# A maximum over partitions taken on another engine, the sums of a weight moved ahead of one tile, and four loads moved behind a loop

## What is computed

```python
# 1: 4 sequences, 8 heads, 768 steps, head size 64: a decaying state
state = gamma * state + outer(k[t], v[t]);  y[t] = scale * q[t] @ state
# 2: x is y as (3072, 512); phi has 32 columns (slots), 4 of them for each of 8 experts
logits = x @ phi
d = softmax(logits, axis=0)              # over the 3072 rows: a maximum and a sum by column
slot_in = (d.T @ x).reshape(8, 4, 512)
slot_out[e] = relu(slot_in[e] @ w1[e]) @ w2[e]
x2 = softmax(logits, axis=1) @ slot_out
# 3: x2 (3072, 512): each row goes to its two best of 8 experts
out[rows] += weight * (relu(x2[rows] @ w1b[e]) @ w2b[e])
```

## Time and profile before

| | |
|---|---|
| median of 3 runs | 539.45 us (538.11 to 540.13) |
| the profiled execution | 539.68 us, its span 537.8 us |
| busy in the span | PE 492.4 us, PEld 291.5, DVE 276.2, ACT 185.8, POOL 254.2 |
| DMA | 107.93 MB, mean 201 GB/s |
| chain that ended last | PE 76%, DMA 13%, DVE 3%, issue 3% |

### The profile page before, as it was taken

The page is one execution under the profiler, slowest core; times in us unless marked ns, Lnnn a source line. Parts: engine busy times, 40 slices in busy tenths (PEclk is TensorE's granted clock), DMA queues, the critical chain, the costliest instruction groups (busy, mean ns, idle before and its releaser), DMA issues.

```text
span 537.8 us, 13565 instructions
## 1 busy us (share of the span) xinstructions
PE 492.4 (92%) x4844; PEld 291.5 (54%) x4845; DVE 276.2 (51%) x443; ACT 185.8 (35%) x346; POOL 254.2 (47%) x217
## 2 busy tenths in 40 slices
PE   3999999987978667989999999999999999999995
PEld 3877787863567243444544544545545445445452
DVE  2676766666221897463646455464545332433422
ACT  0222222221003537665455363554442222223210
POOL 2222222202000024525777868786878766666553
PEclk9999999998997889999999999999999999999999
DMA  7999999989999999342466342132232332433410
GB/s 276 400 359 398 401 401 404 380 340 333 403 425 424 390 417 400 112 174 85 161 217 198 102 137 49 27 58 45 44 59 44 53 47 43 57 42 42 60 20 2
DMA packets 35096, 107.93 MB, mean 201 GB/s; under 512 B 11871, under 2 KB 13135, under 8 KB 32624
## 3 DMA queue, kind: packets, MB, share of 16 engines
q1 hardware_dynamic: 20880, 92.90, 44.6%
q0 software_dynamic: 14176, 14.49, 14.8%
HBM read 93.87 MB, written 29.43 MB: 229 GB/s over the span
## 4 chain that ended last, share of the span: by engine, by line
PE 76%; DMA 13%; DVE 3%; issue 3%; POOL 2%; ACT 1%; SPq 1%; DVEq 0%; POOLq 0%
PE ps L1019 47%; DMA w_region<-moe_w 7%; PE ps L1002 4%; PE ps L672 4%; PE ps L736 4%; DMA late_w1a<-chunks 4%; PE ps L856 3%; PE ps L885 3%; DMA out<-s_region,rec_region 2%; PE ps L712 2%; PE ps L726 2%; PE ps L747 2%; PE ps L686 1%; POOL out L625 1%; SPq L524 1%
## 5 line engine op out<-in xcount | busy, mean ns | idle before, releaser
L1019 PE MATMUL ps<-w_region,s_region 128*128 (+1 forms) x1304 | 290.4, 379 | 2.0 <-DVE s_region L1704 1.0
L1019 PEld LDWEIGHTS ps<-w_region,s_region 128*128 128x128 f16 x1304 | 125.4, 98 | 143.4 <-issue 2.8
L1674 DVE SCALAR_TENSOR_TENSOR s_region<-ps,s_region 128x1024 f16<-128x1024 f32 x55 | 67.3, 1224 | 144.2 <-ACT s_region L1232 144.1
L1232 ACT ACTIVATE s_region<-ps 128x1024 f16<-128x1024 f32 x55 | 56.3, 1024 | 176.5 <-PE ps L1002 176.5
L619 POOL DMA_INDIRECT out<-s_region,rec_region x41 | 53.9, 1315 | 49.4 <-DVE s_region L1704 46.1
L625 POOL DMA_INDIRECT out<-s_region,rec_region x42 | 66.9, 1593 | 19.2 <-issue 11.9
L613 POOL DMA_INDIRECT rec_region<-records,idx x55 | 60.1, 1092 | 24.4 <-issue 16.3
L559 POOL TENSOR_TENSOR s_region<-w_region,s_region 128x512 f32<-128x512 f32 x14 | 14.6, 1043 | 50.0 <-PE ps L747 31.9
L1002 PEld LDWEIGHTS ps<-s_region,sw_region 128*128 (+1 forms) x440 | 29.6, 98 | 14.0 <-issue 0.8
L1704 DVE TENSOR_SCALAR s_region<-ps,rec_region,y_scale 128x512 f32<-128x512 f32 x42 | 33.8, 805 | 5.9 <-PE ps L1019 4.1
L1002 PE MATMUL ps<-s_region,sw_region 128*128 128x128 f16 x440 | 34.5, 219 | 0.5 <-ACT s_region L1227 0.4
(11 more groups left out here) (249 smaller groups left out, 571.1 us busy)
## 6 DMA issues: line engine op xcount, KB each, us to landing
w_region<-moe_w SPq DMA_DIRECT2D x49, 512.0 KB, 11.2
w_region<-moe_w SPq DMA_DIRECT2D x10, 2048.0 KB, 8.7
w_region<-chunks SPq DMA_DIRECT2D x26, 512.0 KB, 7.2
s_region<-moe_w SPq DMA_DIRECT2D x4, 2048.0 KB, 12.9
sw_region<-chunks SPq DMA_DIRECT2D x12, 512.0 KB, 7.2
late_w1a<-chunks SPq DMA_DIRECT2D x8, 512.0 KB, 8.2
w_region<-moe_w SPq DMA_DIRECT2D x3, 1024.0 KB, 8.0
s_region<-moe_w SPq DMA_DIRECT2D x5, 512.0 KB, 8.4
```

Source lines behind the costliest of these rows:

```text
L1019: last = nc.tensor.matmul(bank[6 + r], h[:, r, f, :], w2b_parts[:, bass.ds(o, 1), part, f, :].rearrange("p e m -> p (e m)"), start=(first ...
L1232: nc.scalar.activation(h_hi[:, r, :, :].rearrange("p c t -> p (c t)").rearrange("p (a n) -> p a n", a=2), ps[:, 2 + 2 * r:4 + 2 * r, :], A ...
L1674: nc.vector.scalar_tensor_tensor(out=h_lo[:, r, :, :].rearrange("p c t -> p (c t)").rearrange("p (a n) -> p a n", a=2), in0=ps[:, 2 + 2 * ...
```

## The change

1. **Pieces of w1a.** 26 of the 30 early pieces are issued between the chunks instead of all, and later: one with each of chunks 3 to 10, then four with every three chunks. The other four (the second half of expert 6 and the first of expert 7) are issued behind the noise, ahead of the wait for the last chunk's result; PE waits for them at expert 6.
2. **The last group's maximum.** DVE joins its maximum over chunks with the maximum so far, which still stands spread in PSUM, and POOL reduces these 32 columns over the partitions in one instruction; DVE subtracts the result (shift_last). The old way by PE stays for the fade, behind that. POOL makes one such reduction of ones before it, which nothing reads. spread_max of the last group is gone.
3. **Slots turned and summed in one step.** Four matmuls with the stacked identity (128x32) take the place of four transposes and DVE's sum over four parts; DVE zeroes in_blocks before find_max, where POOL did.
4. **w2b's second half-sum.** ACT takes both sums of the second expert ahead of the Relu of tile 1, POOL reduces them between the record fetches 5 and 6, and DVE makes the scales before the low part of tile 1 and the result of tile 0.

On ACT, where tile 1's Relu stands among the sums of w2b: before,

The diff without its semaphores and the plain renumbering of one wait:

```diff
@@ -69,6 +70,7 @@
+        CHUNK_QUARTERS = EARLY_QUARTERS - 4
@@ -213,6 +214,8 @@
         rec_src_f = rec_src_flat.bitcast(F32).rearrange("p (k t w) -> p k t w", k=2, t=NT)
+        last_max = rec_region[:, 1700:1700 + SL].bitcast(F32)
+        first_reduced = rec_region[:, 1740:1740 + SL].bitcast(F32)
         rec_pad = sb("rec_pad", [1, RW], I32)
@@ -457,23 +463,23 @@
-            def w1a_quarter(e, q):
+            def w1a_quarter(e, q, full):
                 words = slice(q * UNIT // 4, (q + 1) * UNIT // 4)
                 to = late_w1a if e == E - 1 else w1a_home[e]
-                sp.dma_start(to[:, words], w1a[e, :, words]).then_inc(w1a_early, 16)
+                sp.dma_start(to[:, words], w1a[e, :, words]).then_inc(full, 16)
             ahead = 0
             for g in range(3, NT):
                 load_qk(g)
                 load_kv(g)
-                more = (g - 2) * EARLY_QUARTERS // (NT - 3)
+                more = g - 2 + max(0, g - 8) // 3
                 for q in range(ahead, more):
-                    w1a_quarter(q // 4, q % 4)
+                    w1a_quarter(q // 4, q % 4, w1a_early)
                 ahead = more
                 if g == NC:
                     sp.dma_start(gates[:, :, 0:E], w_gate.rearrange("(c p) e -> p c e", p=P)).then_inc(small_full, 16)
                     sp.dma_start(gates[:, :, E:2 * E], w_noise.rearrange("(c p) e -> p c e", p=P)).then_inc(small_full, 16)
-            assert ahead == EARLY_QUARTERS
+            assert ahead == CHUNK_QUARTERS
@@ -532,6 +538,8 @@
             sp.dma_start(noise_t, noise[:, :, :]).then_inc(noise_full, 16)
+            for q in range(CHUNK_QUARTERS, EARLY_QUARTERS):
+                w1a_quarter(q // 4, q % 4, w1a_late)
             sp.wait_ge(x_t_ready, NT)
@@ -589,8 +597,9 @@
-            pool.wait_ge(x_turned, NT)
-            nc.gpsimd.memset(in_blocks, 0.0).then_inc(blocks_zeroed, 1)
+            nc.gpsimd.partition_all_reduce(first_reduced, ones[:, 0:SL], P, MAX)
+            pool.wait_ge(group_max_ready, 1)
+            nc.gpsimd.partition_all_reduce(last_max, col_max[:, 0, :], P, MAX).then_inc(last_max_ready, 1)
             pool.wait_ge(slot_in_done, NG)
@@ -633,7 +642,10 @@
             sw_all_sum(*SW_GROUPS[2])
-            for i in range(4, 2 * DEPTH + 3):
+            for i in range(4, DEPTH + 2):
+                fetch_records(i)
+            w2b_all_sum(EARLY)
+            for i in range(DEPTH + 2, 2 * DEPTH + 3):
                 fetch_records(i)
@@ -647,8 +659,6 @@
                     fetch_records(i + DEPTH + 2)
-                if i == 0:
-                    w2b_all_sum(EARLY)
                 for o in FIRST:
@@ -832,20 +842,22 @@
             den_sums(NG - 2, NT)
-            spread_max(NG - 1)
             slot_sums(NG - 1, range(REP), bank[1], NT)
             den_sums(NG - 1, NT)
             pe.wait_ge(slot_in_kept, NG)
             for d in range(DC):
-                last = nc.tensor.transpose(bank[4][:, d * P:(d + 1) * P], slot_acc[:, d * P:(d + 1) * P], ident[:, :])
+                last = nc.tensor.matmul(bank[4][:, d * SL:(d + 1) * SL], slot_acc[:, d * P:(d + 1) * P], stack,
+                                        start=(d == 0), stop=(d == DC - 1), skip_group_check=True)
             last.then_inc(slot_in_turned, 1)
             pe.wait_ge(slot_in_ready, 1)
             pe.wait_ge(den_kept, NG)
-            pe.wait_ge(w1a_early, 16 * EARLY_QUARTERS)
+            pe.wait_ge(w1a_early, 16 * CHUNK_QUARTERS)
             for e in range(E):
                 w = w1a_home[e].rearrange("p (c f) -> p c f", c=DC)
+                if e == CHUNK_QUARTERS // 4:
+                    pe.wait_ge(w1a_late, 16 * (EARLY_QUARTERS - CHUNK_QUARTERS))
                 if e == E - 1:
@@ -1109,6 +1121,8 @@
                 nc.scalar.activation(exp_of(g), exp_of(g), ACT.Exp).then_inc(exp_cols_ready, 1)
+                if g == NG - 1:
+                    act.wait_ge(max_diag_ready, NG)
                 if g > 0:
@@ -1249,14 +1263,13 @@
             sw_keep(14)
-            w2b_sum_part(EARLY, 0, junk)
             stage_c(2, 0, rec_arrival(2))
+            w2b_sums(EARLY, junk)
+            keep_ct(2, 0)
             h_high(1, 1)
-            keep_ct(2, 0)
             stage_c(3, 1, rec_arrival(3))
+            keep_ct(3, 1)
             h_high(2, 0)
-            keep_ct(3, 1)
-            w2b_sum_part(EARLY, 1, junk)
             w2b_high(EARLY)
@@ -1325,6 +1338,10 @@
                                              AX_X, ALU.max))
+                if g == NG - 1:
+
+                    nc.vector.tensor_tensor(col_max[:, 0, :], col_max[:, 0, :], spread_at, ALU.max).then_inc(group_max_ready, 1)
+                    dve.wait_ge(group_max_ready, 1)
                 nc.vector.tensor_copy(col_max[:, 1:REP, :], col_max[:, 0:1, :].to_broadcast([P, REP - 1, SL])
@@ -1332,6 +1349,10 @@
                 link(nc.vector.tensor_reduce(found[:, g:g + 1], turned_at, AX_X, ALU.max))
+                if g == NG - 1:
+                    nc.vector.tensor_tensor(max_all[:, g:g + 1], max_new[:, g:g + 1], max_all[:, g - 1:g],
+                                            ALU.max).then_inc(max_diag_ready, 1)
+                    return
                 if g > 0:
@@ -1339,9 +1360,15 @@
+            def shift_last():
+                dve.wait_ge(last_max_ready, 1)
+                nc.vector.tensor_tensor(exp_last, logits[:, GROUPS[-1][0]:GROUPS[-1][1], :],
+                                        last_max.unsqueeze(1).to_broadcast([P, REP, SL]),
+                                        ALU.subtract).then_inc(cols_shifted, 1)
+
             def shift_cols(g):
                 dve.wait_ge(max_spread, g + 1)
-                if 0 < g < NG - 1:
+                if g > 0:
@@ -1417,18 +1444,16 @@
+            link(nc.vector.memset(in_blocks, 0.0))
             find_max(NG - 1)
+            shift_last()
             join_max(NG - 1)
-            shift_cols(NG - 1)
             join_slots(NG - 2)
             join_slots(NG - 1)
             dve.wait_ge(slot_in_turned, 1)
-            link(nc.vector.tensor_reduce(slot_in_t[:, :, :], bank[4][:, :].rearrange("p (c j s) -> p c s j", c=DC, j=REP),
-                                         AX_X, ALU.add))
-            dve.wait_ge(blocks_zeroed, 1)
             block_in = in_blocks.rearrange("p (e z) -> p e z", z=in_step)[:, :, 0:DC * SL]
             nc.vector.tensor_copy(block_in.rearrange("p e (c y) -> p e c y", c=DC)[:, :, :, 0:SE],
-                                  slot_in_t[:, :, :].rearrange("p c (e s) -> p e c s", e=E)).then_inc(slot_in_ready, 1)
+                                  bank[4][:, 0:DC * SL].rearrange("p (c e s) -> p e c s", c=DC, e=E)).then_inc(slot_in_ready, 1)
             nc.vector.tensor_copy(same.rearrange("p (j s) -> p j s", j=REP), stack.unsqueeze(1).to_broadcast([P, REP, SL]))
@@ -1709,11 +1734,11 @@
-            low_keep(0, 0, None)
-            h_low(2, 0)
             w2b_scale_by_sum(EARLY)
             dve.wait_ge(order_ready, 1)
             scale_y(EARLY)
+            low_keep(0, 0, None)
+            h_low(2, 0)
             w2b_low(EARLY)
             keep_y(1, 1, None)
             for i in range(2, UNROLLED):
```

7 lines of the change are left out of this document (5 added, 2 removed).

## The result

The changed kernel took 541.27 us (median of 20 runs, 539.96 to 548.61) beside 539.7 us for the kernel before (20 runs, 536.6 to 541.59): ratio 1.0048, 95% interval 1.0032 to 1.0064. It is slower by about 0.5% (the two medians lie 0.3% apart); 536.3 us had been forecast. The profiled execution took 541.27 us, its span 539.2 us.

A forecast was written before the change was run, and what follows sets the result against it. The DMA queue was taken to bound the kernel until w1b's last weights, then PE's tiles. Profiled 539.68 - 2.5 (ahead of the tiles) - 0.9 (first tiles) = 536.3 us, chance 0.60; range 534.2 to 539.7.

The forecast's parts named there:

- the queue gains 4.5 - 1.0 - 1.0 = 2.5 us: DMA queue around the loop's end: filling the 4.5 us hole, less 1.0 undone work and 1.0 restart, gains 2.5 us.
- So it runs dry before L529: ... 1.0 us of work is not done there: Before the load at L529: 40.1 MB issued, 40.5 MB movable by 107.4 us, so 0.4 MB, 1.0 us, is lost.
- rival A: Sequence loop: with fewer pieces the queue starves and the 4.5 us only move; only the tiles gain, 538.8 us; chance 0.12.
- its bound of 0: Lower bound of the queue's gain: 0 us if it starves at several places of the loop.
- x = 2.5 us for 32 columns: Last group's maximum: POOL's 32-column reduction takes 2.5 us, bounds 0.4 and 9.3, making the subtraction 1.0 us late.
- Rivals B and D: Last maximum: B, POOL late, x = 6.3, 542.8 us, chance 0.10; D, reduction takes 3.9 us, 538.0 us, chance 0.08.
- Slots, 0.9 us: Turning and summing slots: a dropped 0.7 us reduction and 0.2 us from the matmuls gain 0.9 us.
- the four matmuls have a quarter of the columns, 0.2 us: Turning of slots on PE: four matmuls with fewer columns save 0.2 us.
- The second half-sum, "-0.9 us": First tiles: w2b's sums ahead of tile 1's Relu gain 0.9 us, bounds +0.7 and -2.0.
- The rows' transfers then hang less far back, and DVE's result of tile 4 ... is what is late next: Stop before 251.58 us: DVE's tile 4 result, ending at 247.6, sets it next, so PE goes on at 250.7.
- Rival C: First tiles: Relu late, row write still collides with w2b's next load; +0.7 instead of -0.9, 537.9 us; chance 0.10.
- POOL's wait with the first write behind it: POOL waits until 220.8 us for the sums; last fetch ends at 227.8; tile 4's result covers a cost up to 6 us.

The follow-up runs named there:

- three kernels on one chip: The change with POOL's reduction of w2b's second order ahead of its wait for tile 1's rows, with 26, 28 or 30 pieces: 538.58, 534.63, 537.62 us.
- the first part alone: Kernel before with only the w1a pieces changed (26 in the loop, spread later, four behind): 544.35 us, ratio 0.9981.
- the change on the chip at 544.9 us: The unaltered change, run again on a chip where the kernel before takes 544.9 us: 542.28 us, ratio 0.9948.
- the two cures: Edits to the change: POOL's reduction of w2b's second order ahead of the landing wait (538.36 us), or w2b's load for order 3 later (538.26 us).

## Why the prediction was wrong

*The pieces, "the queue gains 4.5 - 1.0 - 1.0 = 2.5 us".* The failed step is "So it runs dry before L529: ... 1.0 us of work is not done there". The hole closed and PE's chunk waits went, as said. But the loop lost 3.2 us of transfer in the change, and 351 to 365 GB/s is what all eight profiles with 26 pieces show, against 371 to 381 in the eight with 30. I had assumed the old rate up to the point where the supply ends; it was lower from 40 us on. The term measured 0.64 us in the profile instead of 2.5. This is rival A's outcome, and its bound of 0 is what three kernels on one chip bear out (26 pieces against 30: +1.0 us, the intervals overlap). Its mechanism, a queue standing dry, explains a part only: the DMA share fell from 0.990 to 0.974 in the mean of the eight profiles each, the rate by 5%.

*The last maximum, x = 2.5 us for 32 columns.* It took 0.43. The line through 1 and 3 columns had taken scatter for a slope: reductions of 1 and 2 columns take 0.37 to 0.41 us, and 0.9 right behind a row addition, while the same one of 3 columns took 0.54 us in the kernel before, 0.38 with the first part alone and 1.68 in the change. POOL's start of 9.36 us was near the 8.7 taken. DVE's zeroing lay in DVE's wait, as I had placed it; it cost 0.06 us at most. Between maximum and subtraction 1.35 us were gained where 1.0 had been taken as lost. The subtraction came at 121.46, 1.2 us before the forecast 122.7, the first product at 125.88 (forecast 126.1, with a loop 1.1 us later than I had it). The estimate of 3.9 us made from the GPSIMD Engine Reference of the Trainium skill (§3.2, Cross-partition) doesn't hold for this operation: the row has 0.43. Rivals B and D had no ground.

*Slots, 0.9 us.* The failed step is "the four matmuls have a quarter of the columns, 0.2 us": they took 1.08 us instead of 0.66, not 0.2 less. From the end of DVE's last join of the slots to the first product it is 1.51 us instead of 1.75, a gain of 0.24; between the subtraction and that join 0.34 us were lost. Parts 2 and 3 together still shorten the chain by 1.2 us, where -1.0 + 0.9 was forecast; that the first product came near the forecast is luck, two errors that cancel. Since the queue ends later, little of it arrives.

*The second half-sum, "-0.9 us".* Up to tile 6 this was right and even too careful. In the times of before, 0.64 us later than those of the change, the Relu came at 220.8 (forecast 221.0) and PE's stretch of 40 at 222.7 (forecast 222.8). The waits of 0.69 and 0.99 us went, and 1.6 us were gained where I had 0.3. The failed step is "The rows' transfers then hang less far back, and DVE's result of tile 4 ... is what is late next". I moved the chain of the next stop with PE's lead. Its releaser is a landing that does not move with it: tile 1's rows were issued 2.1 us sooner (232.68 for 234.76), but the addition behind their landing started only 0.3 us sooner (243.09 for 243.42), since they share the DMA engines with a 2 MB load that the same lead also brings forward. So the whole lead turned into waiting, and in two of the four profiles with such a stop the clock fell behind it and took 1.5 to 1.7 us more. The term measured +2.0 us instead of -0.9, in the profile: PE went on at 251.26, only 0.3 us sooner than before where w1b had been 0.6 sooner, and the clock took 1.7. Without the clock it is +0.3 here, +0.5 in the run with the pieces as before, and +1.4 in the change on the chip at 544.9 us; the last two are counted from the end of w1b's last product, against the profile of the kernel before, which is of another run. Rival C named this very collision and priced it at +0.7, the late Relu alone, where it costs the lead and the clock as well. With one of the two cures, ten profiles have 325.9 to 327.0 us of tile part: half-sum and cure together are worth 1.3 to 2.4 us against the 328.3 before. The cure without the half-sum wasn't run.

*POOL's wait with the first write behind it.* The last fetch ended at 227.08 (forecast 227.8), the write followed at 227.39 and took 2.12 us, and its cover held.

*The range.* It ended at 539.7; 541.3 was outside it. A and C came together, with C's price too low: the upper end was A with half of C, and even A with the whole of C, at my prices, gives 540.4. On another chip the change is 0.5% faster. Why the sign turns there isn't shown: ACT's late Relu in the kernel before, seen in traces of two other such chips, would explain it; the trace of before, taken on a chip without it, could not show it.
